# Gated attention in chunks of 64 tokens instead of 128, ahead of two feed-forward networks

## The chip, the cores and the metric

The kernel runs on one NeuronCore of a Trainium2 chip. The metric is the device time of one execution in microseconds (us).

## The reference

```
# attention: batch 4, 8 heads, 768 tokens, head_dim 48, all fp32
f = 1.0 / (1.0 + np.exp(-f_logit))
for t in range(S):
    state = f[:, :, t, :, None] * state + np.einsum('bhd,bhe->bhde', k[:, :, t], v[:, :, t])
    y[:, :, t] = np.einsum('bhd,bhde->bhe', q[:, :, t], state)
x = y as (3072 tokens, 384)
x = (x @ w_a) * (x @ w_b) @ w_out                     # d_ff 1536
p = domain_probs / (domain_probs.sum(-1, keepdims=True) + 1e-09)
out = sum over 4 e: p[:, e:e + 1] * (np.maximum(x @ w1[e], 0.0) @ w2[e])   # 1024 columns each
```

## The kernel before, in words

The recurrence is computed in chunks. Within a chunk, the sum of the log decays from the chunk's start is taken (c), queries are multiplied by exp(-c) and keys by exp(c). Then y of a chunk is (masked scores of the chunk) times v, plus the state ahead of the chunk times q; the state goes from chunk to chunk by a multiplication with the chunk's whole decay and an addition of k v.

Two heads (a pair) stand side by side on partitions 0 to 47 and 64 to 111 (P2 = 112). A unit is a pair and half of the 768 tokens, UT = 384: three chunks of CH = 128. There are NU = 32 units, in groups of four pairs (PPB = 4): units 0 to 3 are the first halves of four pairs, 4 to 7 their last halves, and so on. half_of(u) tells which. The last chunk of a pair needs no k v, so chunks(u) is 2 in last halves, and no state stands ahead of the first chunk.

A unit passes through these steps, each a function on one engine, which is given the unit and waits on semaphores:
- VectorE limit, ACT logs (Exp, Ln), VectorE sums (one scan for each chunk, L1344), ACT decays and inverses (Exp to dec and to the unit), VectorE ends (cend, the decay at each chunk's end, L1348), GpSimd gates (q and k times these, L1177, L1179; VectorE does some of it in the first four units).
- VectorE keys (gated keys times the chunk's whole decay, to kr, L1374), TensorE turn (transposes, L1812), ACT evac_krt (to krt, L920).
- TensorE scores (L1829): for each chunk and head, keys and queries of 48 rows; the two heads lie in the two row halves of the array. VectorE mask (L1387): copies the scores where causal is 1 into att, which holds zeros elsewhere.
- TensorE kv (L1844; in the first four units L1850, both heads in one matmul). VectorE state (L1410 to L1423): the chain over the chunks, into st_in and st_carry, from k v in PSUM.
- TensorE output: state times q (L1868: both heads at once, 112x112, with zeros outside the heads' blocks; L1872 in the first four units, 48x48 blocks), then scores times v (L1880), all added up in one PSUM bank. ACT evac_y (L928, L929) copies y out, and for one unit in four SyncE's store_x moves parts of it on (L752).

All of this is fp32. The products of the two feed-forward networks are fp32r matmuls of 384 columns, three for each product (high and low parts). up_1 and down_1 (L1885 to L1887) are the first network, and the later lines the second.

The order is written out by hand on every engine. The first four units (FIRST = 4) stand ahead of the matmuls of the network, in two sets of PSUM banks (SETS, by two(u)), with a few idle matmuls (L1953) between them. The other 28 are spread over the loop over j, the steps of the first network (three for each of its 96 tiles: up a, up b, down): J[u] is the step at which turn(u) stands, and the tables such as TOGETHER add to it the distance of each other step. They come 5 steps apart up to unit 7 and 6 from there on, so that output(u), kv(u+1) and scores(u+1) mostly stand behind each other. ACT and VectorE run the same loop, with the parts of the network (a_out, h_round, gate, h_rest) and, in its first 27 steps, the splitting of the weights (split_hi, first_lo) as its pieces are loaded.

## Time and profile before

| what | |
|---|---|
| median of 3 runs | 1313.09 us (1311.73 to 1408.94) |
| span of the profiled execution | 1310.4 us |
| TensorE busy | 1301.5 us, 99% |
| VectorE busy | 825.4 us, 63% |
| ACT busy | 622.0 us, 47% |
| GpSimd busy | 549.4 us, 42% |
| granted TensorE clock, mean | 1.000 |

The profile is of one execution, and its span is the time from the first to the last instruction. PE is TensorE's matmuls, PEld its weight loads, which overlap them, DVE is VectorE, POOL GpSimd, SP SyncE. Each fp32 matmul of two passes has two MATMUL rows. The duration of a matmul contains its way through the array, so the durations of matmuls that follow each other overlap; the spacing is read from the starts. A form such as "48*128 48x128" is rows and columns of the weights, then the moving operand.

### The profile page before, as it was taken

The numbers are of one execution on the slowest core, as the hardware profiler recorded it, in microseconds if no ns is written. First come the engines' busy times: TensorE is split into PE (matmuls) and PEld (weight loads), VectorE is DVE, ScalarE is ACT, GpSimd is POOL, SyncE is SP. The second block draws the span as 40 slices with busy tenths as digits, with TensorE's granted clock in tenths as the row PEclk, the third lists the DMA queues.
The fourth block names the chain that finished last, engine by engine and source line by source line (L and its number), as shares of the span: only waits on it lengthen the run. The fifth ranks groups of instructions, "written<-read, shape, count | busy, mean of one in ns | idle before, by whom it ended". The sixth has DMA issues, their size and how long they took to land.

```text
span 1310.4 us, 23459 instructions
## 1 busy us (share of the span) xinstructions
PE 1301.5 (99%) x8223; PEld 1278.5 (98%) x8223; DVE 825.4 (63%) x1678; ACT 622.0 (47%) x1259; POOL 549.4 (42%) x560
## 2 busy tenths in 40 slices
PE   8999999999999999999999999999999999999998
PEld 7999999999999999999999999999999999999998
DVE  7855554555433324367777777777677776777765
ACT  7654544444432323354545554545544455544442
POOL 3321211212135856234445644446544447444441
PEclk9999999999999999999999999999999999999999
DMA  8512122122204343132332343322343313343211
GB/s 253 157 59 60 54 62 60 53 62 61 62 1 144 99 140 125 31 97 80 96 97 72 91 136 91 89 91 69 107 125 96 95 63 93 98 131 98 87 60 49
DMA packets 71686, 117.59 MB, mean 90 GB/s; under 512 B 7120, under 2 KB 49808, under 8 KB 71568
## 3 DMA queue, kind: packets, MB, share of 16 engines
q1 hardware_dynamic: 71568, 116.08, 29.4%
q8 instruction: 67, 1.10, 0.4%
q14 instruction: 51, 0.42, 0.1%
HBM read 102.94 MB, written 14.55 MB: 90 GB/s over the span
## 4 chain that ended last, share of the span: by engine, by line
PE 97%; DVE 1%; DMA 1%; SPq 0%; issue 0%; ACT 0%; DVEq 0%
PE bank L1885 12%; PE bank L1887 11%; PE bank L1886 11%; PE bank L2119 10%; PE bank L2120 10%; PE bank L2121 10%; PE bank L2013 8%; PE bank L2015 8%; PE bank L2014 8%; PE bank L1829 2%; PE bank L1880 2%; PE bank L1868 1%; PE bank L2091 1%; PE bank L2090 1%; PE bank L2089 1%; PE bank L1812 1%
## 5 line engine op out<-in xcount | busy, mean ns | idle before, releaser
L1270 POOL TENSOR_TENSOR wu<-w_r,wu 128x640 fp32r<-128x640 f32 (+1 forms) x132 | 200.6, 1522 | 315.1 <-ACT wu L954 315.1
L2119 PE MATMUL bank<-wd,h_hi 128*128 128x384 f32 x768 | 259.8, 338 | 0.5 <-issue 0.3
L2120 PE MATMUL bank<-wd,h_hi 128*128 128x384 f32 x768 | 257.6, 335 | 0.0
L2121 PE MATMUL bank<-wd,h_lo 128*128 128x384 f32 x768 | 257.1, 335 | 0.0
L1678 DVE SCALAR_TENSOR_TENSOR xt<-bank,pn,xt 128x384 f32<-128x384 f32 x288 | 177.2, 615 | 101.0 <-PE bank L2121 91.7
L981 ACT ACTIVATE h_hi<-h 128x384 fp32r<-128x384 f32 x240 | 124.6, 524 | 193.4 <-DVE h L1628 81.5
L2015 PE MATMUL bank<-x_lo,wu 128*128 128x384 f32 x600 | 202.6, 338 | 0.0
L2013 PE MATMUL bank<-x_hi,wu 128*128 128x384 f32 x600 | 201.4, 336 | 0.0
L2014 PE MATMUL bank<-x_hi,wu 128*128 128x384 f32 x600 | 200.8, 335 | 0.0
L1885 PE MATMUL bank<-xs_hi,wab 128*128 128x384 f32 x570 | 196.8, 345 | 1.4 <-ACT a_sb L992 1.4
L1886 PE MATMUL bank<-xs_hi,wab 128*128 128x384 f32 x570 | 191.2, 335 | 0.0
L1887 PE MATMUL bank<-xs_lo,wab 128*128 128x384 f32 x570 | 191.0, 335 | 0.0
L1275 POOL TENSOR_TENSOR wd<-raw,wd 128x384 fp32r<-128x384 f32 x128 | 133.3, 1056 | 88.0 <-ACT wd L959 84.3
L1649 DVE SCALAR_TENSOR_TENSOR h_lo<-h,h_hi 128x384 fp32r<-128x384 f32 x240 | 135.7, 580 | 50.2 <-ACT h_hi L981 45.0
L969 ACT ACTIVATE h<-bank 128x384 f32<-128x384 f32 x200 | 97.6, 490 | 146.3 <-PE bank L2015 143.8
L1445 DVE TENSOR_TENSOR h_sb<-a_sb,bank 128x384 f32<-128x384 f32 x96 | 53.2, 554 | 162.5 <-PE bank L1887 160.9
L2119 PEld LDWEIGHTS bank<-wd,h_hi 128*128 128x128 f32 x768 | 144.1, 188 | 5.9 <-DVE xt L1678 4.4
L2120 PEld LDWEIGHTS bank<-wd,h_hi 128*128 128x128 f32 x768 | 144.3, 188 | 0.0
L2121 PEld LDWEIGHTS bank<-wd,h_lo 128*128 128x128 f32 x768 | 144.2, 188 | 0.0
L1177 POOL TENSOR_TENSOR unit<-unit,dec 112x384 f32<-112x384 f32 x28 | 30.9, 1103 | 223.9 <-ACT dec L909 223.9
L992 ACT ACTIVATE a_sb<-bank 128x384 f32<-128x384 f32 x96 | 47.3, 493 | 146.8 <-PE bank L1887 146.8
L2013 PEld LDWEIGHTS bank<-x_hi,wu 128*128 128x128 f32 x600 | 112.6, 188 | 2.5 <-DVE h L1608 1.0
(158 smaller groups left out, 2406.2 us busy)
## 6 DMA issues: line engine op xcount, KB each, us to landing
w_r<-weight_sums SPq DMA_DIRECT2D x120, 320.0 KB, 2.9
raw<-w SPq DMA_DIRECT2D x48, 576.0 KB, 3.9
unit<-fkq SPq DMA_DIRECT2D x28, 504.0 KB, 4.2
v_in<-v_chunks SPq DMA_DIRECT2D x32, 144.0 KB, 3.9
out<-xt SPq DMA_DIRECT2D x24, 192.0 KB, 4.4
weight_sums<-w_s SPq DMA_DIRECT2D x10, 384.0 KB, 4.4
weight_sums<-w SPq DMA_DIRECT2D x40, 64.0 KB, 2.7
raw<-w SPq DMA_DIRECT2D x6, 384.0 KB, 3.2
```

The source lines that it names most:

```text
L1270: eng.tensor_tensor(wu_piece(g, n, 1), wu_raw(g, n), wu_piece(g, n, 0).bitcast(f32), ALU.subtract).then_inc(s_ulo, 1)
L1649: eng.scalar_tensor_tensor(out=h2_lo[:, g % 2, o, :], in0=h2[:, o, :], scalar=0.0, in1=h2_hi[:, g % 2, o, :].bitcast(f32), op0=ALU.max, op ...
L1678: eng.scalar_tensor_tensor(out=acc(b, t), in0=d, scalar=w, in1=acc(b, t), op0=ALU.mult, op1=ALU.add).then_inc(s_acc, 1)
L1885: eng.matmul(o, w_hi, m_hi, start=start, stop=False)
L1886: eng.matmul(o, w_lo, m_hi, start=False, stop=False)
L1887: return eng.matmul(o, w_hi, m_lo, start=False, stop=stop)
L2013: eng.matmul(to, w_hi, x_hi, start=start, stop=False, skip_group_check=True)
L2014: eng.matmul(to, w_lo, x_hi, start=False, stop=False, skip_group_check=True)
L2015: eng.matmul(to, w_hi, x_lo, start=False, stop=True, skip_group_check=True).then_inc(s_step, 1)
L2119: eng.matmul(o, hh, w_hi, start=(f == fs[0]), stop=False)
L2120: eng.matmul(o, hh, w_lo, start=False, stop=False)
L2121: mm = eng.matmul(o, hl, w_hi, start=False, stop=(f == fs[-1]))
```

## The change

CH is 64 and CPU (chunks per unit) 6; TPU = 3 counts the blocks of 128 tokens. All units take the same path.
- sums is one scan over all 384 tokens, of which a row "reset" (1, and 0 at every chunk's start) cuts the chunks apart, and then a minimum with CMAX.
- scores: 12 matmuls instead of 6, 64x64 each. Odd chunks write the upper 64 partitions, so a unit uses all four 64x64 tiles of the array (rows by head, columns by the chunk's parity). mask copies only the blocks of 64x64 on the diagonal, in two instructions of 64 partitions (one for each parity) with 2 x 3 x 64 elements.
- kv: 12 matmuls (10 in last halves), 64 rows by parity and columns by head; the results stand in the two banks of the scores, behind their 192 columns. In the first four units kv(u) now waits for mask(u), and output(2) stands ahead of kv(3).
- state: 5 or 6 instructions of 112x48, each of which waits for the one ahead of it; st_first is gone, the zeros outside the blocks too.
- output: scores times v first (unchanged matmuls of 128 tokens), then state times q in 12 (10) matmuls of 48x48 weights and 64 columns, on the diagonal tiles.
- turn: three transposes in all units, and krt is copied whole. turn of the first four waits for the krt two units ahead instead of the state.

```diff
-    CH = 128
-    CPU = 3
+    CH = 64
+    CPU = 6
+    TPU = UT // 128
...
             def sums(u):
+                c = unit_ring[ring(u)][0:P2, F, :]
                 eng.wait_ge(s_log, u + 1)
-                for cc in range(CPU):
-                    c = unit_ring[ring(u)][0:P2, F, cc * CH:(cc + 1) * CH]
-                    eng.tensor_tensor_scan(c, c, cmax[0:P2, :], 0.0, ALU.add, ALU.min).then_inc(s_cum, 1)
+                eng.tensor_tensor_scan(c, reset[0:P2, :], c, 0.0, ALU.mult, ALU.add).then_inc(s_scan, 1)
+                eng.wait_ge(s_scan, u + 1)
+                eng.tensor_scalar(c, c, CMAX, None, ALU.min).then_inc(s_cum, 1)
...
-                for cc in range(CPU):
-                    if half_of(u) == UPP - 1 and cc == CPU - 1:
-                        return
+                for cc in range(chunks(u)):
...
+                    new, old, kv = st_after(u, cc)[0:P2, :], st_before(u, cc)[0:P2, :], kv_place(u, cc)[0:P2, :]
+                    if half_of(u) == 0 and cc == 0:
+                        eng.tensor_copy(new, kv).then_inc(s_st, 1)
+                    else:
+                        eng.scalar_tensor_tensor(out=new, in0=old, scalar=cend[0:P2, g:g + 1], in1=kv,
+                                                 op0=ALU.mult, op1=ALU.add).then_inc(s_st, 1)
...
+                src = unit_ring[ring(u)]
+                for cc in range(CPU):
+                    c, side = cc // 2, cc % 2
+                    for h, start in enumerate((0, 64)):
+                        o = SCORE_BANKS[two(u)][64 * side:64 * side + CH, h, c * CH:(c + 1) * CH]
+                        mm = eng.matmul(o, src[start:start + D, K, tokens(cc)], src[start:start + D, Q, tokens(cc)],
+                                        start=True, stop=True, tile_position=(start, 64 * side))
...
+                else:
+                    eng.wait_ge(s_mask, 2 * (u + 1))
                 for cc in range(chunks(u)):
...
+                    c, side = cc // 2, cc % 2
+                    rows = slice(64 * side, 64 * side + CH)
+                    for h, start in enumerate((0, 64)):
+                        width = 64 if h == 0 else D
+                        a, d = c * P2 + start, (c * 2 + h) * D
+                        mm = eng.matmul(kv_place(u, cc)[start:start + width, :], krt[rows, a:a + width],
+                                        v_in[rows, u % VRING, d:d + D], start=True, stop=True,
+                                        tile_position=(64 * side, start))
...
+                for cc in range(1 - half_of(u), CPU):
+                    for start in (0, 64):
+                        mm = eng.matmul(o[start:start + D, tokens(cc)], st_before(u, cc)[start:start + D, :],
+                                        unit_ring[ring(u)][start:start + D, Q, tokens(cc)], start=False, stop=True,
+                                        tile_position=(start, start), skip_group_check=True)
...
-            kv(3)
             output(2)
+            kv(3)
             output(3)
```

TensorE, between two parts of the first network, at units of last halves (before: state times q, scores times v, kv, scores; the size is that of the result):

```order
L1868 MATMUL bank<-unit,st_carry 112x128
L1868 MATMUL bank<-unit,st_in 112x128 x2
L1880 MATMUL bank<-att,v_in 48x128 x6
L1844 MATMUL bank<-v_in,krt 48x48 x4
L1829 MATMUL bank<-unit 128x128 x6
```
and after the change (scores times v, state times q, kv, scores; the two L1843 rows stand there five times in turn):

```order
L1859 MATMUL bank<-att,v_in 48x128 x6
L1864 MATMUL bank<-unit,st_carry 48x64 x2
L1864 MATMUL bank<-unit,st_in 48x64 x10
L1843 MATMUL pair<-v_in,krt 64x48
L1843 MATMUL pair<-v_in,krt 48x48
...
L1823 MATMUL pair<-unit 64x64 x12
```
Scores times v has moved ahead of the state's part, and each of the other groups has two or more times as many matmuls, of half the columns.

TensorE at the end of the first four units, from scores(3) on, before (scores, kv(3), output(2), output(3)):

```order
L1829 MATMUL bank<-unit 128x128 x6
L1850 MATMUL bank<-v_in,krt 112x96 x3
L1872 MATMUL bank<-unit,st_first 48x128 x4
L1880 MATMUL bank<-att,v_in 48x128 x6
L1872 MATMUL bank<-unit,st_first 48x128 x4
L1880 MATMUL bank<-att,v_in 48x128 x6
```
and after (scores(3), output(2), kv(3), whose two rows stand there six times, output(3)):

```order
L1823 MATMUL pair<-unit 64x64 x12
L1859 MATMUL pair<-att,v_in 48x128 x6
L1864 MATMUL pair<-unit,st_in 48x64 x10
L1843 MATMUL pair<-v_in,krt 64x48
L1843 MATMUL pair<-v_in,krt 48x48
...
L1859 MATMUL pair<-att,v_in 48x128 x6
L1864 MATMUL pair<-unit,st_in 48x64 x10
```
kv(3) stands behind output(2) now.

VectorE in the first four units, from mask(0) over ends, keys, state(0) and ends to the sums, before:

```order
L1387 COPY_PREDICATED att<-causal,bank 128x384 x2
L1348 COPY cend<-dec 112x3
L1374 TENSOR_TENSOR kr<-unit,cend 112x384
L1410 COPY st_first<-bank 112x96
L1412 SCALAR_TENSOR_TENSOR st_first<-st_first,cend,bank 112x96
L1423 SCALAR_TENSOR_TENSOR st_carry<-st_first,cend,bank 48x48 x2
L1348 COPY cend<-dec 112x3
L1344 SCALAR_TENSOR_TENSOR unit<-unit,cmax 112x128 x3
```
and after:

```order
L1397 COPY_PREDICATED att<-causal,pair 64x6x64 x2
L1356 COPY cend<-dec 112x6
L1382 TENSOR_TENSOR kr<-unit,cend 112x384
L1412 COPY st_in<-pair 112x48
L1414 SCALAR_TENSOR_TENSOR st_in<-st_in,cend,pair 112x48 x4
L1414 SCALAR_TENSOR_TENSOR st_carry<-st_in,cend,pair 112x48
L1356 COPY cend<-dec 112x6
L1350 SCALAR_TENSOR_TENSOR unit<-reset,unit 112x384
L1352 TENSOR_SCALAR unit<-unit 112x384
```
The chain of the state has six instructions instead of four, and the sums two instead of three.

## Rows read from the trace of the kernel before

**Rows 1.** The page, parts 1 and 4: busy time by engine; engines of the last chain.

```profile
PE 1301.5 (99%) x8223; PEld 1278.5 (98%) x8223; DVE 825.4 (63%) x1678; ACT 622.0 (47%) x1259; POOL 549.4 (42%) x560
...
PE 97%; DVE 1%; DMA 1%; SPq 0%; issue 0%; ACT 0%; DVEq 0%
```

**Rows 2.** Lines and forms, TensorE, 0 to 700 us: count | busy us, mean ns | idle.

```profile
L1868 PE MATMUL bank<-unit,st_in 112*112 112x128 f32 x112 | 16.8, 272 | 0.0
L1812 PE MATMUL bank<-ident,kr 112*128 112x112 f32 x80 | 13.0, 260 | 0.5 <-DVE kr L1374 0.5
```

**Rows 3.** Time order, TensorE, 102.7 to 105.3 us: start us, lasting us, what, passes.

```profile
102.64 0.60 PE L1868 MATMUL bank<-unit,st_in 112*112 112x128 f32 x4
103.17 0.86 PE L1880 MATMUL bank<-att,v_in 128*48 128x128 f32 x12
103.87 0.44 PE L1844 MATMUL bank<-v_in,krt 128*48 128x48 f32 x12
104.23 0.94 PE L1829 MATMUL bank<-unit 48*128 48x128 f32 x12
105.10 0.45 PE L1885 MATMUL bank<-xs_hi,wab 128*128 128x384 f32 x1
```

**Rows 4.** Time order, TensorE, narrow windows: only the passes in them.

```profile
103.65 0.39 PE L1880 MATMUL bank<-att,v_in 128*48 128x128 f32 x4
...
104.04 0.26 PE L1844 MATMUL bank<-v_in,krt 128*48 128x48 f32 x4
...
97.66 0.45 PE L1812 MATMUL bank<-ident,kr 112*128 112x112 f32 x3
```

**Rows 5.** Time order, TensorE, in the first four units, narrow windows.

```profile
15.76 0.42 PE L1872 MATMUL bank<-unit,st_first 48*48 48x128 f32 x4
...
23.46 0.36 PE L1850 MATMUL bank<-v_in,krt 128*112 128x96 f32 x2
```

**Rows 6.** Lines and forms, TensorE's weight loads, 0 to 700 us.

```profile
L1880 PEld LDWEIGHTS bank<-att,v_in 128*48 128x48 f32 x384 | 19.4, 122 | 4.4 <-issue 0.7
L1868 PEld LDWEIGHTS bank<-unit,st_in 112*112 112x112 f32 x112 | 14.9, 175 | 0.0
```

**Rows 7.** Time order, VectorE, 5 to 32 us.

```profile
7.48 0.33 DVE L1338 TENSOR_SCALAR unit<-unit 112x384 f32<-112x384 f32 x1
7.74 1.06 DVE L1344 TENSOR_TENSOR_SCAN unit<-unit,cmax 112x128 f32<-112x128 f32 x3
...
14.32 0.25 DVE L1410 COPY st_first<-bank 112x96 f32<-112x96 f32 x1
14.60 0.31 DVE L1412 SCALAR_TENSOR_TENSOR st_first<-st_first,cend,bank 112x96 f32<-112x96 f32 x1
14.95 0.56 DVE L1423 SCALAR_TENSOR_TENSOR st_carry<-st_first,cend,bank 48x48 f32<-48x48 f32 x2
15.54 0.17 DVE L1348 COPY cend<-dec 112x3 f32<-112x3 f32 x1
...
17.74 1.07 DVE L1387 COPY_PREDICATED att<-causal,bank 128x384 f32<-128x384 int32 x2
18.71 0.24 DVE L1410 COPY st_first<-bank 112x96 f32<-112x96 f32 x1
...
25.29 1.34 DVE L1436 TENSOR_TENSOR xs_lo<-xt,xs_hi 128x384 fp32r<-128x384 f32 x1
```

**Rows 8.** TensorE after the first stretch; windows: length, busy PE, PEld, DVE, ACT, POOL, clock, DMA.

```profile
31.34 0.45 PE L1885 MATMUL bank<-xs_hi,wab 128*128 128x384 f32 x1 [1.36 <-ACT a_sb L992]
...
8.00:26.00 18.00, 16.30 (x186) 13.40 (x186) 17.05 (x47) 14.74 (x29) 9.40 (x7) 1.00 0.86 261
52.00:56.00 4.00, 4.00 (x25) 4.00 (x24) 3.90 (x10) 2.38 (x5) 0.00 (x0) 1.00 0.86 260
```

**Rows 9.** Time order, 0 to 60 us: the matmuls that only warm up.

```profile
1.59 7.26 PE L1953 MATMUL bank<-ident 128*128 128x128 f32 x42 [1.59 <-POOL ident L1160]
...
11.06 1.52 PE L1953 MATMUL bank<-ident 128*128 128x128 f32 x12
```

More of the change, by code:

```diff
@@ L637, in states @@
         def states(u, n):
-            def some(x, chunks):
-                return sum(1 if x < FIRST and cc < CPU - 1 else 2 for cc in range(chunks))
-            return sum(some(x, CPU if half_of(x) < UPP - 1 else CPU - 1) for x in range(u)) + some(u, n)
+            return sum(chunks(x) for x in range(u)) + n
         def is_strong(eng):
@@ L919, in evac_krt @@
                     eng.wait_ge(s_kv, u)
[L920 removed]
+                eng.activation(krt[:, :], SETS[two(u)][0][:, 0:TPU * P2], ACT.Copy).then_inc(s_krt, 1)
             def evac_y(u):
@@ L1808, in turn @@
                 elif before_in_two(u) >= 0:
-                    eng.wait_ge(s_st, states(before_in_two(u) + 1, 0))
+                    eng.wait_ge(s_krt, before_in_two(u) + 1)
                 o = SETS[two(u)][0]
-                for cc in range(chunks(u)):
-                    mm = eng.transpose(o[:, cc * P2:(cc + 1) * P2], kr[two(u)][0:P2, cc * CH:(cc + 1) * CH],
+                for c in range(TPU):
+                    mm = eng.transpose(o[:, c * P2:(c + 1) * P2], kr[two(u)][0:P2, c * 128:(c + 1) * 128],
                                        ident[0:P2, 0:P2])
@@ L1972, in _ @@
             scores(3)
+            output(2)
             kv(3)
-            output(2)
             output(3)
```

152 lines of the change are left out of this document (55 added, 97 removed).

## The prediction

> **What bounds the kernel now.** The page comes first. It shows a TensorE that is busy 99% of the span and holds 97% of the chain of work that ended last [rows 1]. So an edit counts for what it does to TensorE's own stream, and wherever TensorE waits. The chain leaves TensorE only in the first 31 us, where the first four units run with nothing else to do. There VectorE is busy 17.05 of 18 us from 8 to 26 [rows 8], and the last of that waiting is a TensorE idle of 1.36 us at 31.34 for ACT's a_sb [rows 8]. From then on the attention steps of the other 28 units are inserted into an unbroken matmul stream, and each nanosecond that they gain or lose is one of the span.
>
> So the view by line and form comes next, for the counts [rows 2], and then the time order of one unit, for the real spacing [rows 3]. The mean durations are no guide there: an fp32 matmul is two passes (two MATMUL rows each), and their tails overlap. What counts is start to start.
> - L1868 (112x112 weights, 128 columns): four passes take 0.60 of which the last is 0.272 [rows 2, 3], so 0.109 each.
> - L1880 (two column halves, 128 columns): its last four passes last 0.39 [rows 4], and one, like L1868's, 0.27. That leaves 0.12 for all their steps. The trace shows them as pairs: 0.11 from pair to pair and under 0.01 within one, two tiles in the time of one.
> - L1829 (two row halves, 128 columns): 12 in 0.94 [rows 3]; less the last 0.27 and 0.10 for a change of form (below) that is 0.57 over five steps, 0.11 again.
> - L1844 (two column halves, 48 columns): 12 passes in 0.44 and four in 0.26 [rows 3, 4], so 0.18 for four more pairs, 0.045 each.
> - L1872 of the first units (48x48 tiles on the diagonal): four passes in 0.42 [rows 5], the last 0.27, so 0.15 from the first pair to the second, of which some 0.04 is the start of a new form.
>
> 128 columns at 0.109 and 48 at 0.045 are 0.8 ns a column and some 4 ns, whatever the tile, and what lies in different tiles overlaps. Weights can bound it as well: L1850 (112 weight columns, only 96 moving) takes 0.10 a pass (two in 0.36 with a tail of 0.26) [rows 5], where its columns would take 0.08. The loads of 48 and of 112 columns take 122 and 175 ns [rows 6], so 0.8 ns for each weight column too: the period is the longer of the two counts times 0.8 ns and about 5 ns more. A change between tile forms costs besides: from L1868's last start (102.64 + 3 x 0.109 = 102.97) to L1880's first is 0.20 instead of 0.11, and L1829 is followed by a pass that is 0.45 long instead of 0.34 [rows 3].
>
> **The TensorE stream after the change, per unit of the 28 behind the first four.** Three changes of form stand in such a group before and after (into 128x64, onward, back), so they cancel.
> - Scores: 6 matmuls (6 pairs of passes, 6 x 0.11 = 0.67) become 12 over four 64x64 tiles with 64 columns: 24 passes, four at once, 6 periods of 64 x 0.8 + 5 = 57 ns = 0.34. Gain 0.33.
> - k v: 6 or 4 matmuls (0.27 or 0.18) become 12 or 10 over the four tiles; half have 64 weight columns, so by the weight count 58 ns a period: 6 or 5 periods, 0.35 or 0.29. Loss 0.08 (whole unit), 0.11 (last half).
> - The state's part of y: 2 or 3 full matmuls (4 or 6 passes, 0.44 or 0.66) become 10 or 12 in the two diagonal tiles, 10 or 12 periods of 57 ns: 0.57 or 0.68. Loss 0.13 or 0.03.
> - The transposes: 3 in all units, where units of the last half had 2. Three of L1812 take 0.45 with a tail of 0.26 [rows 2, 4], so 0.095 each. Loss 0.095 there.
> - Scores times v: unchanged.
>
> The 12 units of first halves gain 0.33 - 0.08 - 0.13 = 0.11 each, the 16 of last halves 0.33 - 0.11 - 0.03 - 0.095 = 0.09 each: **2.8 us less** in all. No row has four tiles at once. From below, a group of four could do no better than the periods above. From above, if a pass can start no closer to the next than in the nearest row, L1844's average of 22.5 ns, the groups are longer (first rival); if tiles did not overlap at all, far longer (second).
>
> **The other engines in the stream.** VectorE per unit: one scan of 384 and one minimum for three scans. A minimum is 0.33 as L1338 is, three scans 1.06 [rows 7]; one scan saves two starts and walks as many elements, 0.8 to 1.06. I take 0.9, so +0.26 with the starts that overlap. The state chain is 5 or 6 instructions of 112x48 that each wait for the last. The 0.35 from the start at 14.60 to that at 14.95, for an instruction of 0.31 [rows 7], makes a waiting step its duration and 0.04; at L1423's 0.26 that is 0.30, so 1.5 to 1.74, up to 0.5 more than now. Together +0.75 of VectorE a unit. It is covered: the busiest stretch, 52 to 56 us with the weight splits, has it at 3.90 of 4 [rows 8], but the results are due one to two steps later, and TensorE waits for none of them now. I put 0 in the sum and up to 2 us in the range. ACT's wider copy of the transposes (112 more columns, about 0.1) is covered: ACT is busy 47% [rows 1].
>
> **The first four units.** This stretch has no cover, VectorE's order decides, and there are three additions there.
> - Sums: +0.26 in each of four, 1.0.
> - State: 14.32 to 15.54 is 1.22 for four instructions [rows 7]; a copy at 0.24 and five waiting steps at 0.30 are 1.74. +0.52 each, 2.1 in all.
> - k v now waits for its own unit's mask. Until now it ran while VectorE masked: the state of unit 1 starts at 18.71, the moment the mask from 17.74 is through [rows 7]. Afterwards, mask, then the change of form 0.1, six periods 0.35 and about 0.2 until the last pass is there: 0.65 to 0.7. In unit 0 the ends and keys between mask and state cover it. Units 1 and 2 have nothing between them, 0.7 each. For unit 3 the new order puts output(2) ahead: it waits for state(2), lasts some 1.5 (0.67 + 0.57, two changes of form and the tail), then k v 0.7, against the mask's 0.97 that runs meanwhile: 1.25.
>
> Sum: 1.0 + 2.1 + 0.7 + 0.7 + 1.25 = 5.75, so x_first_lo(0), at 25.29 now, starts at about 31. Not all of it reaches the stream. The 1.36 idle before 31.34 is ACT held up by late weight loads (two splits stand ahead of a_sb); these loads move only by what the first y is late (output(0) from 15.76 [rows 5] to about 16.9, so 1.2), and are there in time afterwards. Followed through ACT: output(3) ends near 32.5, y out 1.0, x1_hi 0.5, two splits 1.7, a_sb 0.5: TensorE goes on at about 36.2 instead of 31.34, **4.9 us later**. If the scan is as cheap as it can be and k v is covered better, 3; with the mask's strided reads or the scan at the dear end, 8.
>
> **The sum** against the profiled span: 1310.4 + 4.9 - 2.8 = 1312.5. The median of the runs is 1313.1, which is 2.7 over the profiled span, so 1315.2 as a timed run. A change of 2% is 26 us, about what a measurement of this kernel can tell from none.
>
> **Rivals.**
> - *Small passes have a floor.* If passes of different tiles cannot average closer than L1844's 22.5 ns [rows 3, 4], scores take 0.54, k v 0.54 or 0.45: a unit is 0.27 longer than now instead of 0.1 shorter, 28 x 0.27 = 7.4, and with 4.9 the time is 1325.4. For it: no row shows more than two tiles at once. Against it: the members of a pair start under 10 ns apart, so issue itself is not the 22.5. The Trainium skill ("TensorE: Matmul & The Clock Gate", the section on 56 ns and 53.3 ns) states a stronger form, start to start never under about 25 ns; by that, scores would be 0.60 and k v 0.60 or 0.50, and the estimate 1329. The pairs in L1844 at 22.5 on average are already under it. 0.18.
> - *Four tiles don't overlap* (slower). Then the groups of scores and k v run pass by pass, at 57 and about 50 ns: 1.37 and 1.2 or 1.0, and the state tiles, which write one bank, likewise 1.14 or 1.37. A unit is 1.7 longer, 28 x 1.7 = 48, time 1366. It becomes slower by 2% from 0.76 us a unit on (21.3 / 28). Against it: L1829, L1844 and L1872 each overlap two tiles. The Trainium skill ("TensorEngine Tiling (Array Packing)", Gotcha 1) says that different row tiles cannot access one PSUM bank at the same time, which speaks against the diagonal tiles of y. L1872 does just this, and its pairs take 0.11 like the rest, so the trace disagrees. 0.06.
> - *The clock falls in the first units.* TensorE will wait up to 1.9 us at a time there, at some 60% work. At the start of the trace 42 passes of L1953 last 7.26 us, where 12 later ones take 1.52 [rows 9]: less the tail 0.17 against 0.11 a pass, so much of that time was at 1.2 GHz. If the stream began as cold as that, some 5 us at half pace cost 2.5: 1318. Now it doesn't fall with waits of 1 us. 0.08.
> - *The head is hidden*: loads and ACT's queue were what held 31.34, and the new order overlaps better than I follow it. Then 1310 to 1312, the 2.8 visible. Against it: VectorE has no room from 8 to 26 us [rows 8]. 0.08.
>
> **How the numbers follow.** My forecast has 0.60, with its own range 1311 to 1321 (head 3 to 8, stream -4 to +1). The range 1310 to 1330 takes in the floor, the clock and most of the hidden head; 0.06 for no overlap and some 0.08 at the edges stay out. Slower by over 2% is the second rival and a tail of several costs together, 0.07. Faster by over 2% would need 1 us a unit, more than the scores cost in all: 0.01. Within 2%: 0.92.
>
> **What would show it.** In the new trace: scores as fours that start within 0.03, at about 0.057 a four, some 0.35 between the first k v of a group and the first score; y's state passes in pairs at 0.057; the first wide matmul of the stream after a_sb at 36 instead of 31.3; the state of units 1 and 2 idle 0.7 for k v. The forecast is wrong if the wide stream's start moves by under 3 or over 8 us, if fours show starts 22 ns or more apart, or if rows of the stream wait for VectorE's gate or state.

## The result, and the profile after

| | before | after |
|---|---|---|
| median of 11 runs | 1312.46 us | 1315.18 us |
| lowest | 1310.98 us | 1313.45 us |
| span of the profiled execution | 1310.4 us | 1311.7 us |
| granted TensorE clock, mean | 1.000 | 0.998 |
| VectorE busy | 825.4 us | 850.5 us |

The ratio is 1.0027, with a 95% interval from 1.0019 to 1.0035: slower by 2.5 to 4.6 us, which is far under 2%. The forecast was 1315.2. The profiled execution shows a difference of only 1.3 us. The 11 runs of after spread over 5.2 us (1313.45 to 1318.67), and the profile is of the quickest. One run of before took 1408.94 us and is not counted in the ratio.

The page of after, parts 1 and 4 (answers to [rows 1]):

```profile
PE 1297.0 (99%) x9559; PEld 1269.7 (97%) x9559; DVE 850.5 (65%) x1672; ACT 621.1 (47%) x1259; POOL 549.5 (42%) x558
...
PE 97%; DVE 1%; issue 0%; DMA 0%; ACT 0%; POOL 0%; SPq 0%; DVEq 0%; POOLq 0%
```

TensorE has 1336 more passes and is busy 4.5 us less. It is the bound as before, and the first 36 us are again where it is not.

Time order of TensorE after the change: the waits of the head and its low-clock stretch, then one group of the stream (start us, lasting us, what, passes, idle ahead and who ended it):

```profile
20.20 0.56 PE L1843 MATMUL pair<-v_in,krt 64*64 64x48 f32 x24 [1.95 <-DVE att L1397]
...
22.40 0.92 PE L1823 MATMUL pair<-unit 48*64 48x64 f32 x24
...
26.37 0.58 PE L1823 MATMUL pair<-unit 48*64 48x64 f32 x24 [0.40 <-ACT xt L938]
...
31.30 0.86 PE L1859 MATMUL pair<-att,v_in 128*48 128x128 f32 x12 [1.94 <-DVE st_carry L1414]
...
36.48 0.45 PE L1870 MATMUL bank<-xs_hi,wab 128*128 128x384 f32 x1 [0.78 <-ACT a_sb L1001]
...
45.85 0.41 PE L1870 MATMUL bank<-h_hi,wo_hi 128*128 128x384 f32 x1 [0.66 <-DVE h_lo L1440]
...
107.57 0.34 PE L1872 MATMUL pair<-h_lo,wo_hi 128*128 128x384 f32 x1
107.83 0.86 PE L1859 MATMUL bank<-att,v_in 128*48 128x128 f32 x12
108.63 0.70 PE L1864 MATMUL bank<-unit,st_in 48*48 48x64 f32 x17
109.12 0.24 PE L1843 MATMUL pair<-v_in,krt 64*48 64x48 f32 x1
...
109.47 0.27 PE L1823 MATMUL pair<-unit 48*64 48x64 f32 x2
...
109.51 0.57 PE L1823 MATMUL pair<-unit 48*64 48x64 f32 x22
110.01 0.44 PE L1870 MATMUL bank<-xs_hi,wab 128*128 128x384 f32 x1
110.29 0.34 PE L1871 MATMUL bank<-xs_hi,wab 128*128 128x384 f32 x1
```

The same place of before, around the group of [rows 3], shows two wide matmuls that its group stands between:

```profile
102.47 0.34 PE L1887 MATMUL bank<-h_lo,wo_hi 128*128 128x384 f32 x1
...
105.39 0.34 PE L1886 MATMUL bank<-xs_hi,wab 128*128 128x384 f32 x1
```

From the last wide matmul ahead to the second one behind, a group took 105.39 - 102.47 = 2.92 before and takes 110.29 - 107.57 = 2.72 now. The 24 passes of the scores last 0.61 here, from 109.47 to the end of the row at 109.51, of which one pass's own 0.22 is the tail: 0.39 / 23 = 17 ns on average from pass to pass (0.36 in the quickest group, 0.42 in the slowest). In the single starts inside the group the fours follow each other by 0.058.

Time order of VectorE after the change, up to x_first_lo(0) (answers to [rows 7]):

```profile
5.84 0.95 DVE L1350 TENSOR_TENSOR_SCAN unit<-reset,unit 112x384 f32<-112x384 f32 x1
6.83 0.36 DVE L1352 TENSOR_SCALAR unit<-unit 112x384 f32<-112x384 f32 x1
7.10 0.35 DVE L1345 TENSOR_SCALAR unit<-unit 112x384 f32<-112x384 f32 x1
...
11.86 0.97 DVE L1352 TENSOR_SCALAR unit<-unit 112x384 f32<-112x384 f32 x1
12.76 1.18 DVE L1397 COPY_PREDICATED att<-causal,pair 64x384 f32<-64x384 int32 x2
13.97 0.17 DVE L1356 COPY cend<-dec 112x6 f32<-112x6 f32 x1
...
14.84 0.21 DVE L1412 COPY st_in<-pair 112x48 f32<-112x48 f32 x1
15.08 1.16 DVE L1414 SCALAR_TENSOR_TENSOR st_in<-st_in,cend,pair 112x48 f32<-112x48 f32 x4
16.28 0.27 DVE L1414 SCALAR_TENSOR_TENSOR st_carry<-st_in,cend,pair 112x48 f32<-112x48 f32 x1
16.46 0.17 DVE L1356 COPY cend<-dec 112x6 f32<-112x6 f32 x1
...
20.81 0.21 DVE L1412 COPY st_in<-pair 112x48 f32<-112x48 f32 x1 [0.76 <-PE pair L1843]
...
25.61 0.21 DVE L1412 COPY st_in<-pair 112x48 f32<-112x48 f32 x1 [1.00 <-PE pair L1843]
...
29.44 0.21 DVE L1412 COPY st_in<-pair 112x48 f32<-112x48 f32 x1 [0.98 <-PE pair L1843]
...
31.07 0.55 DVE L1427 TENSOR_TENSOR xs_lo<-xt,xs_hi 128x384 fp32r<-128x384 f32 x1
```

Windows of after: length, busy PE, PEld, DVE, ACT, POOL, clock, DMA share, GB/s:

```profile
18.00:20.00 2.00, 0.25 (x10) 0.10 (x4) 1.93 (x4) 1.82 (x4) 1.24 (x2) 1.00 0.85 214
20.00:22.00 2.00, 1.80 (x30) 1.78 (x31) 1.10 (x6) 0.00 (x0) 0.98 (x1) 0.67 0.21 48
22.00:24.00 2.00, 2.00 (x35) 1.59 (x35) 1.71 (x5) 1.49 (x3) 0.67 (x1) 0.50 0.20 49
24.00:26.00 2.00, 1.97 (x55) 1.52 (x51) 0.95 (x3) 1.17 (x3) 2.00 (x2) 0.97 0.44 112
```

The granted clock falls to the level of 1.2 GHz for 3.4 us, from 20.7 to 24.1. It does so behind a stretch in which TensorE worked 0.25 of 2 us. The scores at 22.40 last 0.92 there, and 0.58 at 26.37 at the full clock.

The spread of the runs goes with this clock. Each run has its mean granted clock on record: those of after have 0.991 to 0.998, with spans from 1311.7 us at 0.998 to 1316.5, 1316.6 and 1317.0 us at 0.991, and the median run has 0.994 and 1313.5 us. Before has 0.999 or 1.000 in each of the 18 runs beside experiments 1 and 3 to 5, with spans from 1309.7 to 1311.8 us. So the profiles differ by 1.3 us and the medians by 2.7 us, and most of what lies between goes with a longer stretch at the low clock than the profile of after shows.

**Where the time went.** Three points of the trace settle it. They are the wide matmul that ends the head, which is the 16th of 384 columns in every kernel here, the last wide matmul of the first network, the 2,592nd, and the last of all.

| starts, us | 16th | 2,592nd | between them | last |
|---|---|---|---|---|
| before | 31.34 | 561.34 | 530.00 | 1306.59 |
| after | 36.48 | 562.99 | 526.51 | 1307.97 |
| difference | +5.14 | +1.65 | -3.49 | +1.38 |

The head (all up to the 16th wide matmul) costs 5.14, the stretch with the attention gives back 3.49, and the rest of the kernel is the same to 0.3. I summed the gaps between neighbouring starts over that stretch: those that contain attention matmuls add up to 86.23 before and 82.30 now (-3.93), those from wide matmul to wide matmul to 443.77 and 444.21 (+0.44, among which is the new wait at 45.85). The distance between the two points comes out alike to 0.07 us in every kernel with the same stream, so it serves as the yardstick below, and a 28th of a change in it is that of a unit.

### The profile page after: what moved, and what is told of

Same layout as the page of the kernel before. It is cut to its first block, busy times and chain, and to the rows that moved or that the text cites. A ratio compares the mean times of both kernels' runs of the same rounds, so it can differ in the third digit from the quotient of the medians.

```text
span 1311.7 us, 26134 instructions
## 1 busy us (share of the span) xinstructions
PE 1297.0 (99%) x9559; PEld 1269.7 (97%) x9559; DVE 850.5 (65%) x1672; ACT 621.1 (47%) x1259; POOL 549.5 (42%) x558
## 3 DMA queue, kind: packets, MB, share of 16 engines
q1 hardware_dynamic: 71568, 116.08, 29.3%
## 4 chain that ended last, share of the span: by engine, by line
PE 97%; DVE 1%; issue 0%; DMA 0%; ACT 0%; POOL 0%; SPq 0%; DVEq 0%; POOLq 0%
PE pair L2104 10%; PE pair L2105 10%; PE pair L2106 10%; PE bank L1870 9%; PE bank L1872 9%; PE bank L1871 9%; PE bank L2000 5%; PE bank L1998 5%; PE bank L1999 5%; PE pair L1998 3%; PE pair L2000 3%; PE pair L1999 3%; PE pair L1872 3%; PE pair L1870 3%; PE pair L1871 3%; PE bank L1859 2%
## 5 line engine op out<-in xcount | busy, mean ns | idle before, releaser
L2104 PE MATMUL pair<-wd,h_hi 128*128 128x384 f32 x768 | 259.9, 338 | 0.3 <-issue 0.3
L2105 PE MATMUL pair<-wd,h_hi 128*128 128x384 f32 x768 | 257.6, 335 | 0.0
L2106 PE MATMUL pair<-wd,h_lo 128*128 128x384 f32 x768 | 257.2, 335 | 0.0
L1672 DVE SCALAR_TENSOR_TENSOR xt<-pair,pn,xt 128x384 f32<-128x384 f32 x288 | 177.3, 615 | 100.5 <-PE pair L2106 90.9
L2104 PEld LDWEIGHTS pair<-wd,h_hi 128*128 128x128 f32 x768 | 144.1, 188 | 5.4 <-DVE xt L1672 4.0
L2105 PEld LDWEIGHTS pair<-wd,h_hi 128*128 128x128 f32 x768 | 144.3, 188 | 0.0
L2106 PEld LDWEIGHTS pair<-wd,h_lo 128*128 128x128 f32 x768 | 144.2, 188 | 0.0
L2000 PE MATMUL bank<-x_lo,wu 128*128 128x384 f32 x399 | 134.7, 338 | 0.0
L1998 PE MATMUL bank<-x_hi,wu 128*128 128x384 f32 x399 | 133.9, 336 | 0.0
L1999 PE MATMUL bank<-x_hi,wu 128*128 128x384 f32 x399 | 133.5, 335 | 0.0
L978 ACT ACTIVATE h<-bank 128x384 f32<-128x384 f32 x132 | 64.6, 491 | 97.2 <-PE bank L2000 94.6
L1870 PEld LDWEIGHTS bank<-xs_hi,wab 128*128 128x128 f32 x570 | 106.9, 188 | 3.0 <-ACT a_sb L1001 1.1
```

The lines of the kernel that those rows point to most:

```text
L1672: eng.scalar_tensor_tensor(out=acc(b, t), in0=d, scalar=w, in1=acc(b, t), op0=ALU.mult, op1=ALU.add).then_inc(s_acc, 1)
L1870: eng.matmul(o, w_hi, m_hi, start=start, stop=False)
L1998: eng.matmul(to, w_hi, x_hi, start=start, stop=False, skip_group_check=True)
L1999: eng.matmul(to, w_lo, x_hi, start=False, stop=False, skip_group_check=True)
L2000: eng.matmul(to, w_hi, x_lo, start=False, stop=True, skip_group_check=True).then_inc(s_step, 1)
L2104: eng.matmul(o, hh, w_hi, start=(f == fs[0]), stop=False)
```

## The experiments

All ten are edits of the changed kernel. Two test the tiles, one the changes of form, and seven the head. Each ratio is to the kernel before, timed beside the experiment. Starts, windows and distances are of one profiled execution of each kernel.

**1. Scores over two tiles at a time.** Even chunks first, then odd, so that neighbouring matmuls lie in two tiles instead of four.

```diff
-                for cc in range(CPU):
+                for cc in (0, 2, 4, 1, 3, 5):
                     c, side = cc // 2, cc % 2
```

> The 12 matmuls of the scores stand in another order: the three even chunks first, then the three odd ones, so that only two of the four 64x64 tiles take turns at a time. Nothing else changes. If four tiles really work at once, a group of scores goes from about 0.36 us to twice that (12 periods of 57 ns, 0.68), 28 x 0.33 = 9 us more than the changed kernel, so about 1324. If the short group only came from passes that were short (64 columns), or from a fixed spacing between passes, the order changes nothing: 1315.

Measured: 1319.28 us, ratio 1.0056 (1.0039 to 1.0073); between the two points 531.57, 5.06 more than after. One group, in time order:

```profile
122.73 0.76 PE L1823 MATMUL pair<-unit 48*64 48x64 f32 x24
```

At the median of the 28 groups it is 0.60 from the first start to the last instead of 0.42, so 0.18 a unit and 28 x 0.18 = 5.0. That the use of all four tiles is worth something is confirmed, but only half of what was expected of the order. The rows don't name the tile, but their single starts fall into two series of 12 at 0.058 for each pair: one from 122.73 to 123.08 and one that begins at 122.92, while five passes of the first are still to start. I read them as the even and the odd chunks: matmuls of a free tile are started although earlier ones wait for theirs. The kernel after shows the same more directly: in 28 of its 32 groups of scores, the pass that raises the semaphore, which is the last of the program, is not the last to start. So this experiment did not take the four tiles away entirely. The next one does.

**2. Scores on one side.** Behind the first four units the odd and even chunks write the upper 64 partitions alike, so that two tiles have all the work in any order. Half of the scores overwrite the others, and y is another one; the number and size of all matmuls stay.

```diff
+                        side = 1 if u >= FIRST else side
                         o = SCORE_BANKS[two(u)][64 * side:64 * side + CH, h, c * CH:(c + 1) * CH]
```

> In the 28 units behind the first four, the scores of the even chunks are written to the upper 64 partitions too (over those of the odd ones), so that the scores use two tiles of the array and never four; y is then computed from other scores, the work on every engine is the same in size. With the order changed alone, the tiles of odd chunks still started while the even ones ran, and the group was only 0.16 longer. Here they can't: 12 periods of 57 ns, 0.33 longer than with four tiles, 28 x 0.33 = 9 us more, about 1324. If passes in one tile can overlap as well, it stays under 1320.

Measured: 1323.25 us, ratio 1.0084 (1.0068 to 1.0101); between the points 534.13, 7.62 more than after, 0.27 a unit. In time order:

```profile
112.55 0.27 PE L1824 MATMUL pair<-unit 48*64 48x64 f32 x2
...
112.63 0.84 PE L1824 MATMUL pair<-unit 48*64 48x64 f32 x22
113.39 0.44 PE L1871 MATMUL bank<-xs_hi,wab 128*128 128x384 f32 x1
```

From the first score to the wide matmul it is 0.84 here and 0.54 in after: 0.30 more, near the 0.34 that six periods of 57 ns are. The fours of passes are therefore real, and they are what pays for the scores. The head is 1.85 longer here, though it has the same instructions as in after: the edit starts behind it. What differs is the granted clock, at 0.50 for 10.2 us from 15.2 to 25.4 and again for 3.4 us from 32.3, against 3.4 us in all in after. So 10.2 us more at the low clock went with 1.85 us in this head. The median run of after is 1.8 us over its profiled one, at a mean clock lower by 0.004. Of 1312 us that is 5.2 us, or some 10 us more at half the clock: my estimate, and near the same price.

**3. The state's part first.** This is the order of before: state times q, scores times v, kv, scores.

```diff
+                for cc in range(1 - half_of(u), CPU):
...
                 for c in range(TPU):
...
-                for cc in range(1 - half_of(u), CPU):
...
```

> In output(u) the state's part of y stands first and scores times v behind it, as before the change. The work is the same, but TensorE now goes 64x64, 128x64, 64x64 where it went 128x64, 64x64, 64x64: two changes of form more in each group in which output, k v and scores follow each other (about 24 of 28). At 0.10 to 0.20 us for each change that the trace of before showed, this is 5 to 9 us more, 1320 to 1324. If changes of form cost nothing, and the gaps belong to something else, it stays at 1315.

Measured: 1320.02 us, ratio 1.0057 (1.0041 to 1.0074); between the points 530.25, 3.74 more than after, 0.13 a unit. One group in time order:

```profile
122.69 0.76 PE L1857 MATMUL bank<-unit,st_in 48*48 48x64 f32 x20
123.39 0.86 PE L1864 MATMUL bank<-att,v_in 128*48 128x128 f32 x12
124.18 0.50 PE L1843 MATMUL pair<-v_in,krt 64*64 64x48 f32 x22
124.49 0.26 PE L1823 MATMUL pair<-unit 48*64 48x64 f32 x2
...
125.03 0.45 PE L1870 MATMUL bank<-xs_hi,wab 128*128 128x384 f32 x1
```

In after, state, kv and scores are all 64x64 tiles and stand behind each other, and even their borders overlap: the first kv starts at 109.12, while three of the 20 state passes are still to start. Here scores times v with its 128x64 tiles splits them. Counted from wide matmul to wide matmul that is four changes of form instead of three, one more and not two as I had expected, in the 26 of the 28 units whose output, kv and scores stand together. The gaps that contain attention add up to 86.20 instead of 82.30, so the one change and the border that it takes the overlap from cost 3.90 / 26 = 0.15. The other 2.3 us of this kernel lie in its head, where its clock is at the lower level from 15.3 to 25.6 us and again from 32.4 to 35.8. The Trainium skill ("TensorEngine Tiling (Array Packing)", Key Properties) says that a change of tiling mode drains the TensorE. The trace agrees: at each change in these groups the first pass of the new form starts 0.07 before the recorded end of the last pass of the old one, an end that is modelled (the state's part at 108.63, scores times v until 107.83 + 0.86 = 108.69), while within a form kv starts before the last state pass has.

**4. k v of the first units in other banks.** kv(u) no longer has to wait for mask(u), and kv(3) stands ahead of output(2) again. The idle matmuls write bank 0 instead of 3.

```diff
+            if u < FIRST:
+                return bank[3 + cc % 2][:, a:a + D]
...
-                else:
-                    eng.wait_ge(s_mask, 2 * (u + 1))
+                elif u:
+                    eng.wait_ge(s_st, states(u, 0))
...
+            kv(3)
             output(2)
-            kv(3)
```

> In the first four units k v goes to banks 3 and 4, which nobody reads then, so it no longer waits for its own unit's mask; kv(3) stands ahead of output(2) again, and the idle matmuls write bank 0. If the wait for the mask is what the trace shows before the states of units 1, 2 and 3 (0.76, 1.00 and 0.98 us of idle VectorE), it goes almost whole, and the first wide matmul after a_sb comes 2.3 to 2.7 us earlier (36.5 to about 34): 1312.6. If the chain through output and ACT bounds the head and VectorE's idle only follows it, under 1 us is gained.

Measured: 1311.38 us, ratio 0.9992 (0.9982 to 1.0001); x_first_lo(0) at 28.63 instead of 31.07, the 16th wide matmul at 34.34 instead of 36.48, between the points 526.48 as in after. VectorE's rows at the two state copies that had waited 0.76 and 1.00, with no idle ahead of them:

```profile
20.29 0.21 DVE L1414 COPY st_in<-bank 112x48 f32<-112x48 f32 x1
...
24.13 0.21 DVE L1414 COPY st_in<-bank 112x48 f32<-112x48 f32 x1
```

So the wait for the masks is worth 2.1 to 2.4 us of the head. Without it the rest of the head's loss and the stream's gain cancel, and the kernel is level with before. Its median falls by more, 3.8 us below that of after; its runs have a clock of 0.997 to 0.999 and after's 0.991 to 0.998.

**5. More idle matmuls.** These keep TensorE at work through the waits for the masks: seven more ahead of kv(0), eight ahead of kv(1).

```diff
-            idle(bank[3], AT_KV)
+            idle(bank[3], AT_KV + 7)
...
             output(0)
+            idle(bank[3], 8)
             kv(1)
```

> Seven more idle matmuls ahead of kv(0) and eight ahead of kv(1), where TensorE stood still for 1.7 and 1.95 us; the granted clock fell to the low level from about 20.4 to 23.8 us. If that fall costs time, turn(2), scores(2) and output(1) are through about 1.2 us earlier, the state of unit 2 too, and the whole is 0.7 to 1.2 us shorter: about 1314.2, and the windows show the full clock throughout. If VectorE alone sets the head, the clock is full and the time stays at 1315.2.

Measured: 1315.11 us, ratio 1.0022 (1.0012 to 1.0032), no change. Windows:

```profile
20.00:24.00 4.00, 3.53 (x86) 2.90 (x86) 2.94 (x11) 1.91 (x3) 1.61 (x2) 1.00 0.14 33
...
32.00:36.00 4.00, 4.00 (x28) 3.92 (x23) 3.36 (x7) 2.96 (x5) 0.00 (x0) 0.57 0.26 94
```

The low stretch is gone from 20 to 24 us (x_first_lo(0) starts 0.44 earlier) and stands at 32.5 to 35.9 instead, on the first wide matmuls, where it costs more: the 16th is at 37.19, 0.7 later than in after. From x_first_lo(0) to the 16th it is 5.41 or 5.42 us in after and experiments 1, 6 and 9, whose clock is full there (5.72 in 4), and 6.51 to 6.61 in 2, 3, 5, 7 and 10, which have 3.4 us at the low clock in it: 1.1 to 1.2 us.

**6. Keys behind the masks.** A filler that VectorE has to do anyway is moved to where it waits for kv.

```diff
-            keys(2)
             mask(1)
+            keys(2)
             state(1)
             ends(3)
-            keys(3)
             mask(2)
+            keys(3)
             state(2)
```

> VectorE's keys(2) stands behind mask(1) and keys(3) behind mask(2), in the gap in which VectorE waits for k v (0.76 and 1.00 us). If these gaps are dead time on the path that sets the head, each takes in about 0.45 us of keys, and the first wide matmul comes 0.8 to 1.0 us earlier: about 1314.3. If turn(2) and turn(3), which wait for the keys and stand behind k v on TensorE, become the late ones, nothing is gained.

Measured: 1313.39 us, ratio 1.0011 (1.0001 to 1.0021); x_first_lo(0) and the 16th wide matmul both 1.66 earlier than in after (29.41 and 34.82). VectorE's three waits:

```profile
20.13 0.21 DVE L1412 COPY st_in<-pair 112x48 f32<-112x48 f32 x1 [0.17 <-PE pair L1843]
...
23.96 0.21 DVE L1412 COPY st_in<-pair 112x48 f32<-112x48 f32 x1 [0.34 <-PE pair L1843]
...
27.78 0.21 DVE L1412 COPY st_in<-pair 112x48 f32<-112x48 f32 x1 [0.99 <-PE pair L1843]
```

They are 1.24 shorter together. Of the other 0.42, 0.09 is an earlier first load, and the rest are small waits of VectorE, for the gated keys and for scores(2). Scores(2) lasts 0.76 here and 0.92 in after, where the clock was low; in this profile it did not fall (1.00 in each window from 8 to 36 us). By the starts of VectorE's rows no more than about 0.2 us can be put down to that. The masks come earlier in this order, so TensorE waits for the second one 1.36 instead of 1.95. That this kept the clock up is not shown: five of the ten runs of this kernel have a mean clock of 0.995.

**7. No minimum.** The minimum with CMAX behind the scan is left out. With these inputs it changes nothing, but a step of the computation is missing.

```diff
-                eng.tensor_tensor_scan(c, reset[0:P2, :], c, 0.0, ALU.mult, ALU.add).then_inc(s_scan, 1)
-                eng.wait_ge(s_scan, u + 1)
-                eng.tensor_scalar(c, c, CMAX, None, ALU.min).then_inc(s_cum, 1)
+                eng.tensor_tensor_scan(c, reset[0:P2, :], c, 0.0, ALU.mult, ALU.add).then_inc(s_cum, 1)
```

> The minimum with CMAX behind the scan is left out in all units (with these inputs no sum of 64 log decays reaches CMAX). Prediction's term: it costs 0.27 to 0.33 of VectorE in each unit. In the head all four are on VectorE's path, one of them 0.9 long beside GpSimd's work: the first wide matmul after a_sb comes 1.2 to 1.8 us earlier, and the one wait of TensorE for h_lo behind the head (0.66 us at 45.9) gets shorter or goes, since less work of VectorE stands ahead of it. In all 1.5 to 2.3 us less than the changed kernel: about 1313.3. If the order of the units' waits for TensorE sets the head, the minimum is hidden and nothing moves.

Measured: 1312.77 us, ratio 1.0007 (0.9997 to 1.0017). x_first_lo(0) is 2.08 earlier (28.99), the 16th wide matmul only 0.92 (35.56). The clock fell from 29.3 to 32.8 us, on the last output and the first wide matmuls (0.67 in the window 28 to 32), and the 1.1 to 1.2 us of experiment 5 are the difference. Between the points it is 525.53, 0.98 less than after: the wait for h_lo at 45.85 is gone.

**8. Other banks with idle matmuls.** Experiment 4 with five more idle matmuls behind kv(0) and three ahead of output(0).

```diff
-            idle(bank[0], BETWEEN)
+            idle(bank[0], BETWEEN + 5)
             turn(1)
             scores(1)
+            idle(bank[5], 3)
             output(0)
```

> The kernel with k v in banks 3 and 4 (1311.4), with five more idle matmuls between kv(0) and turn(1) and three between scores(1) and output(0), where TensorE stood for 1.3 and 0.8 us and the clock fell from 16.8 to 20.2 us. If the fall can be kept out of the whole head, output(0), kv(1), turn(2) are early, but VectorE, which has no gap there, sets the pace: 0 to 0.4 us less. If the fall only moves to a later place, as with more idle matmuls in the changed kernel, it costs up to 1 us more when it lands on the first wide matmuls.

Measured: 1312.27 us, ratio 1.0002 (0.9993 to 1.0012). Windows:

```profile
20.00:24.00 4.00, 2.30 (x55) 1.88 (x49) 3.38 (x11) 1.86 (x3) 2.32 (x2) 0.83 0.24 58
24.00:28.00 4.00, 3.66 (x85) 3.04 (x82) 2.82 (x9) 3.33 (x6) 4.00 (x3) 0.50 0.57 152
28.00:32.00 4.00, 4.00 (x50) 3.12 (x48) 2.69 (x9) 2.19 (x5) 0.04 (x1) 0.50 1.05 375
```

In this execution the low clock came 6 us later than in experiment 4's and stayed for 10 instead of 3.4 us, and the 16th wide matmul is 2.3 later. The ten runs have clocks from 0.995 to 1.000, so the stretch is not always that long, and the intervals of the two ratios overlap. The filler is not shown to help.

**9 and 10. The savings together.** The other banks (4) or the moved keys (6), each with the minimum left out (7). The edits are those shown there; of 9 the two that matter:

```diff
-                eng.tensor_scalar(c, c, CMAX, None, ALU.min).then_inc(s_cum, 1)
...
-                    eng.wait_ge(s_mask, 2 * (u + 1))
+                elif u:
+                    eng.wait_ge(s_st, states(u, 0))
```

> The k v of the first four units in banks of their own (as in the kernel with other banks) and the minimum behind the scan left out (it changes nothing with these inputs, but the step is missing from what is computed). Theory, both savings are of different work and add up: 1311.4 of the first less 2.4 of the second, 1309.0, that is 0.9975 of the kernel before; x_first_lo(0) starts near 26.6 (28.63 less 2.08), and no wait for h_lo stands in the stream. Rival, the clock: VectorE's work in the head gets shorter, TensorE's waits with it, so the fall may be gone or be moved into the stream; if it takes 3 us of wide matmuls, they cost 1.5 us more and the time is 1310.5. Rival, ACT: a_sb and the y copies wait for weight loads as in the kernel before, and half of the two savings is not seen: 1311.

> VectorE's keys(2) and keys(3) behind the masks of units 1 and 2, k v in the banks of the scores as changed, and the minimum left out. Theory, additive: after 1315.1 less 1.7 (keys) less 2.4 (minimum) = 1311.0, 0.9990 of before, the first wide matmul behind a_sb near 33.9. Rival, ACT or loads hold the head: no gain over the kernel without the minimum alone, 1312.7.

Measured: 9 has 1307.86 us, ratio 0.9971 (0.9960 to 0.9982), and 10 has 1311.01 us, ratio 0.9989 (0.9980 to 0.9998). The row of 9 that ends its head:

```profile
31.52 0.44 PE L1870 MATMUL bank<-xs_hi,wab 128*128 128x384 f32 x1 [0.77 <-ACT a_sb L1003]
```

In 9 the head ends at 31.52, nearly where it ended before the change (31.34), the clock is at 1.00 in every window, and the stream keeps its gain: 525.54 between the points, 4.46 less than before. That is the whole of the 4.3 by which its span (1306.1) is under that of before. It beats the kernel before by 0.3%, but as it stands only for inputs whose sums stay under CMAX. Of the kernels that compute everything none is shown faster than before; experiment 4 is level with it. It is 1.1 us under the additive 1309.0: x_first_lo(0) comes at 26.10 where 26.6 was expected, and no low stretch takes anything back. In 10, which came out as expected, the clock fell again, at 28 to 32 us (0.57).

| kernel | 16th wide | between the points | median |
|---|---|---|---|
| before | 31.34 | 530.00 | 1312.46 |
| after | 36.48 | 526.51 | 1315.18 |
| 1 two tiles at a time | 36.58 | 531.57 | 1319.28 |
| 2 one side | 38.33 | 534.13 | 1323.25 |
| 3 state's part first | 38.74 | 530.25 | 1320.02 |
| 4 other banks | 34.34 | 526.48 | 1311.38 |
| 5 more idle | 37.19 | 526.53 | 1315.11 |
| 6 keys behind masks | 34.81 | 526.48 | 1313.39 |
| 7 no minimum | 35.56 | 525.53 | 1312.77 |
| 8 banks and idle | 36.64 | 526.46 | 1312.27 |
| 9 banks, no minimum | 31.52 | 525.54 | 1307.86 |
| 10 keys, no minimum | 34.03 | 525.50 | 1311.01 |

The medians are of different sessions. That of before was 1312.46 beside experiments 1 and 3 to 5, 1312.11 beside 2 and 6 to 8, and 1311.81 beside 9 and 10.

## Why the prediction was right, point by point

**The head, VectorE: right in sum, by two errors that cancel.** x_first_lo(0) starts at 31.07 instead of 25.29, 5.78 later where 5.75 was forecast. Each term is read from one start to the next in the time order of VectorE, before and after:

| term | forecast | measured |
|---|---|---|
| sums, four | 1.0 | 1.04 |
| state, four | 2.1 | 1.64 |
| k v waits | 2.65 | 2.74 |
| masks, four | 0 | 1.01 |
| first load there earlier | 0 | -0.67 |

- Sums: a scan and a minimum take 7.10 - 5.84 = 1.26, three scans took 0.97 [rows 7]. One in four is longer in both kernels (1.74 before, 1.89 now). Experiment 7 gets 2.08 back in the head. This is more than the 1.04, because a scan alone takes 0.86 to the next start (as in experiment 9, 9.97 to 10.83): 0.40 less than 1.26 in three units, and 1.03 less than 1.89 in the one with the long minimum (0.97, at 11.86).
- State: 16.46 - 14.84 = 1.62 against 1.22 [rows 7]. The forecast added 0.30 for each of five waiting steps and 0.24 for the copy. The copy (14.84 to 15.08) and four of the steps (15.08 to 16.28) are as forecast. The fifth takes 0.18, since the copy to cend behind it doesn't wait for it: 0.12 too much in each of four units.
- k v: 0.76, 1.00 and 0.98, forecast 0.7, 0.7 and 1.25. Experiment 4 takes them all away, and x_first_lo(0) comes 2.44 earlier.
- Masks: **the term that the sum lacks**. "The mask's strided reads" stood only at the dear end of the range, and nothing in the sum. Two instructions of 64 partitions last 1.18 to 1.22 where two of 128 lasted 1.02 to 1.07 [rows 7], and from start to start it is 13.97 - 12.76 = 1.21 in unit 0, against 0.92; over the four units it is 0.25 each. Both walk 2 x 384 elements a partition, and the new ones in runs of 64. That the runs are the cause was not tested.

**From there to the stream: 5.14, forecast 4.9.** The chain ran through ACT as it was followed, and the 16th wide matmul waited 0.78 for a_sb instead of 1.36.

**The stream: right in direction, too small.** Forecast -2.8, measured -3.49 with the new wait in it; experiments 7, 9 and 10, without that wait, have -4.46 to -4.50. The gaps with attention alone give -3.93. Three terms came as forecast:
- Scores: from the first to the wide matmul it was 105.10 - 104.23 = 0.87 [rows 3] and is 110.01 - 109.47 = 0.54, 0.33 less. Experiments 1 and 2 show that the four tiles pay for this.
- All ahead of k v: 109.12 - 107.57 = 1.55 against 103.87 - 102.47 = 1.40, 0.15 more where the state's part was to cost 0.13.
- The third transpose: the gaps around the transposes grew by 1.53 in all, forecast 16 x 0.095.

The term that was mis-sized is k v. It was to last 0.08 longer in such a group; from its first start to the first score it is 109.47 - 109.12 = 0.35 now and was 104.23 - 103.87 = 0.36. In last halves it grew by 0.05 where 0.11 was forecast. The forecast priced each group by itself, and groups of one form overlap at their borders: the first kv starts while three state passes are still to start, and the first scores start at 109.47, ahead of the last kv at 109.50.

The count of three changes of form, before and after, was right. How much hangs on it shows in experiment 3, which makes it four: 0.15 for each of 26 units takes the whole gain (530.25 between the points against before's 530.00). So smaller chunks pay here only together with the new order of the groups.

**VectorE's work in the stream: forecast 0 with 2 in the range, measured 1.** One row waits for h_lo, 0.66 at 45.85, and 0.98 is what experiment 7 gets back between the points. VectorE at that place, before and after:

```profile
38.00 0.42 DVE L1374 TENSOR_TENSOR kr<-unit,cend 112x256 f32<-112x256 f32 x1 [1.43 <-POOL unit L1179]
...
39.31 0.53 DVE L1449 TENSOR_TENSOR h_lo<-h_sb,h_hi 128x384 fp32r<-128x384 f32 x1
```

```profile
43.48 0.49 DVE L1382 TENSOR_TENSOR kr<-unit,cend 112x320 f32<-112x320 f32 x1 [1.45 <-POOL unit L1186]
...
45.16 0.55 DVE L1440 TENSOR_TENSOR h_lo<-h_sb,h_hi 128x384 fp32r<-128x384 f32 x1
```

It is not that VectorE had no time: it stood idle for 1.45 us for GpSimd just ahead. But keys and sums stand between that wait and h_lo, and they take 45.16 - 43.48 = 1.68 where they took 1.31, mostly for the minimum. The prediction argued from VectorE's busy share, "it is covered"; what counted was the way from GpSimd's result to h_lo. That way is longer by 0.37 here, so it accounts for a part of the 0.66; which steps ahead of GpSimd make up the rest I did not trace.

**The sum.** Against its own profile 1312.5 was forecast and 1311.7 is the span; as a timed run 1315.2, and 1315.18 is the median. The closeness of the latter is luck. The forecast put the 2.7 us between span and median of before on top. In every run on record the time is 1.7 to 1.9 us over the span of the same execution; the rest of the 2.7 was chance between one profile and three runs. For after the distance is 3.5, and the 1.8 beyond the fixed part go with the lower clock of the median run (0.994 against 0.998 in the profile). The forecast had the clock at nothing, with 0.08 for it as a rival. A sum that was 0.8 too high against the profile, and 1.0 of chance in the 2.7, filled the place of those 1.8.

**The rivals.** The floor of 22.5 ns a pass, the first rival, falls: the passes of the scores average 16 to 18 ns from start to start, and 58 ns for four inside a group. So falls the stronger form of the Trainium skill ("TensorE: Matmul & The Clock Gate", the section on 56 ns and 53.3 ns), 25 ns from start to start at least; by that the 24 passes would need 0.58 without a tail, and they start within 0.36 to 0.42. No overlap of four tiles falls by the same row. Its price was also added up wrongly: its own terms, 0.70 for the scores, 0.93 for k v and 0.70 for the state's part in a first half, give 2.3 a unit and not 1.7, so 1383 and not 1366. The state's passes, which write one bank from two row tiles, run in pairs as well: ten pairs in 0.76 with a tail of 0.22, so 0.54 for nine steps, 0.06 each (the 20 passes of experiment 3). The head was not hidden: it is 5.14 longer.

The rival of the clock came true in part. It did not begin the stream cold in the profile of after, but it fell inside the head, and the runs of after have a lower clock than this profile. The head of experiment 2, the same instructions with 10.2 us more at the low clock, is 1.85 longer, and the median run of after is 1.8 longer than its profiled one. Of the 2.7 us between the medians about half is therefore what the instructions cost in the profile, 1.3, and the rest goes with the clock; what a run of after at the full clock throughout would take is not known. Why the clock falls more here than before is not shown. In after TensorE has three waits of 1.7 to 1.95 us in the head and before none above 1.36, but experiment 4 without the waits for the masks still fell, and experiment 6 with them did not in its profile. Nor do the kernels in which kv waits for the masks all spread alike: after, 5, 6, 7 and 10 by 3.6 to 5.2 us, 1 to 3 with four runs each by 1.3 to 3.6, and 4, 8 and 9, without the wait, by 1.6, 3.6 and 1.3.

## What to carry to other kernels

Small fp32 matmuls in different tiles of the array cost the longest tile's queue and not their number, so halving the size can pay on a bound TensorE, if matmuls of one tile form stand beside each other: here one more change of form in a group, 0.15 us, was worth as much as the whole gain. Before a result is put behind another one in a bank to save space, look at what its reader waits for: here that wait alone turned a level kernel into a slower one. Where the bounding engine gains only a tenth of a microsecond a unit, the engine that leads at the start decides, because there the additions have no cover. And two medians a few microseconds apart should be compared with the clock of each run beside them: here it goes with half of the difference.

## What the hardware did that I had not expected

- Matmuls of a free tile start ahead of earlier ones whose tile is taken: with even chunks first, the scores lost 0.18 a unit and not 0.33, and in 28 of 32 groups of after the last matmul of the scores is not the last to start.
- Groups of the same tile form overlap at their borders, by up to three passes of the state's part at 109.12. One more change of form, which also ends such an overlap, cost 0.15 a unit.
- A scan of 384 columns takes 0.95 where three of 128 took 1.05, and the minimum behind it starts 0.99 after it: little is saved by merging them.
- The same head at the low clock for 10.2 us more took 1.85 us more (experiment 2 against after).
- Filling TensorE's waits with idle matmuls did not keep the clock up: in the profiled executions the low stretch stood at 32 us (experiment 5) or was 10 us long (experiment 8). In experiments 6 and 9 there was none, without any filler added, though five of ten runs of 6 have a mean clock of 0.995. What decides it was not found.
